# Normalising and folding the attention output of batches two and three on GpSimd instead of VectorE

## What is computed

```
attention, 4 batches, 8 heads, 576 tokens, 64 wide:
    scores = q @ k.T / 8;  kth = 32nd largest of a row
    attn = softmax(scores where scores >= kth, else -1e9)
    out = attn @ v                       # becomes x, (4, 576, 512)
first block:
    u = x + real(fft over tokens, then over width, of x)
    x = u + relu(norm(u) @ w1) @ w2      # 512 -> 2048 -> 512
second block:
    out = x + relu(norm(x) * g @ w1') @ w2'
```

## Time and profile before

| | us |
|---|---|
| median of 3 runs | 1482.75 (1481.47 to 1484.03) |
| profiled execution | 1480.5, span 1478.7 |
| PE busy | 1323.3 (89%) |
| DVE busy | 1173.6 (79%) |
| ACT busy | 670.9 (45%) |
| POOL busy | 320.0 (22%) |

### The profile page before, as it was taken

How to read it: one execution, slowest core, us unless ns; L and a number is a source line. 1 busy time by engine, 2 the same in 40 slices (tenths; PEclk the granted TensorE clock), 3 DMA queues, 4 the chain that set the end, 5 groups by cost and what they waited for, 6 DMA issues and landing times. The chain is left out here.

```text
span 1478.7 us, 22291 instructions
## 1 busy us (share of the span) xinstructions
PE 1323.3 (89%) x7944; PEld 1054.5 (71%) x7944; DVE 1173.6 (79%) x2345; ACT 670.9 (45%) x1293; POOL 320.0 (22%) x283
## 2 busy tenths in 40 slices
PE   4666768899998799899999899999998999999998
PEld 2434444677676577678877677877887989888887
DVE  7999998799999979999997999854675454555543
ACT  3555543355454335454453464433354434343432
POOL 2443420122131112131220131220123020121210
PEclk9665659999999899899999999999999999999999
DMA  6688770565565426556543454542354343333342
GB/s 209 258 301 312 282 278 9 199 209 201 197 221 185 153 91 212 181 173 195 180 158 120 167 190 150 173 144 70 116 171 140 117 147 117 127 115 123 120 139 76
DMA packets 83295, 248.61 MB, mean 168 GB/s; under 512 B 26417, under 2 KB 26418, under 8 KB 79090
## 3 DMA queue, kind: packets, MB, share of 16 engines
q1 hardware_dynamic: 81554, 241.67, 48.3%
q0 software_dynamic: 1632, 5.51, 1.1%
HBM read 208.34 MB, written 38.27 MB: 167 GB/s over the span
## 5 line engine op out<-in xcount | busy, mean ns | idle before, releaser
L580 PE MATMUL Ac<-wr,hh 128*128 128x512 f32 x1152 | 361.6, 395 | 0.0
L563 PE MATMUL Hp<-uh,wr 128*128 128x256 f32 (+1 forms) x1336 | 305.6, 319 | 7.4 <-ACT hh L763 5.0
L857 DVE MAX8 top<-wk 128x8 f32<-128x576 f32 x432 | 304.5, 746 | 0.0
L563 PEld LDWEIGHTS Hp<-uh,wr 128*128 128x128 f32 x1336 | 225.7, 193 | 55.2 <-issue 47.3
L580 PE MATMUL Ac<-wr,hl 128*128 128x512 f32 x576 | 237.9, 413 | 14.7 <-DVE wr L992 7.5
L580 PEld LDWEIGHTS Ac<-wr,hh 128*128 128x128 f32 x1152 | 218.5, 190 | 40.3
L405 POOL TENSOR_TENSOR hl<-hf,hh 128x256 fp32r<-128x256 f32 (+1 forms) x111 | 96.0, 865 | 537.4 <-ACT hh L763 537.3
L869 DVE MATCH_REPLACE8 wk<-top,wk 128x576 f32<-128x576 f32 x288 | 211.5, 741 | 0.0
L511 PE MATMUL Tp<-ident,ex 128*128 128x128 f32 x720 | 132.2, 317 | 85.4 <-DVE ex L876 81.7
L563 PE MATMUL Hp<-ul,wr 128*128 128x256 f32 (+1 forms) x668 | 206.9, 310 | 0.0
L511 PEld LDWEIGHTS Tp<-ident,ex 128*128 128x128 f32 x720 | 97.7, 162 | 127.5 <-issue 86.9
(11 more groups left out here) (118 smaller groups left out, 1724.5 us busy)
## 6 DMA issues: line engine op xcount, KB each, us to landing
wr<-w_split SPq DMA_DIRECT2D x222, 512.0 KB, 4.8
wf<-in_weights SPq DMA_DIRECT2D x89, 512.0 KB, 3.3
w_split<-wr SPq DMA_DIRECT2D x32, 1024.0 KB, 7.0
sc<-in_weights SPq DMA_DIRECT2D x56, 512.0 KB, 3.2
qT<-in_q SPq DMA_DIRECT2D x16, 288.0 KB, 4.7
kT<-in_k SPq DMA_DIRECT2D x16, 288.0 KB, 5.3
vn<-in_v SPq DMA_DIRECT2D x32, 128.0 KB, 4.9
out<-U POOLq DMA_DIRECT2D x3, 768.0 KB, 6.2
```

Source lines behind the costliest of these rows:

```text
L563: last = nc.tensor.matmul(hidden(n), a[:, kd * P:(kd + 1) * P], x[:, kd, 0:P * SIZE[p]], start=(kd == 0 and j == 0), stop=(kd == KD - 1 an ...
L580: last = nc.tensor.matmul(Ac[:, j, :], a[:, n % 2, j * P:(j + 1) * P], w, start=(f == 0 and m == 0), stop=(f == KF - 1 and m == 2))
L857: nc.vector.max(top[:, s % RING, r, :], src).then_inc(s_top, 1)
```

## The change

For batches 1 and 2 the three stages `normal_x`, `pair_x`, `fold_x` are split. DVE keeps the sums and all work on the 64-row chunk (`sums`, `fold_rest`), now after pair `18(b+1)`, one pair earlier than before. GpSimd gets the norm of the four full chunks in two halves, the two pair sums and the two folds, one of these steps in each of the slots 74 to 79 and 110 to 115, behind its own work on the unit and the turned rows and before residual adds and gains. The pieces of the transform stand two slots later (80 to 84, 116 to 120), and `combined` one pair later. PE's first piece waits for one semaphore more, `s_rem`. `late_exps` lists slots 86, 88, 90 and 122, 124, 126 instead of 74, 76, 84, 86, 88 and 110, 112, 120, 122, 124.

```diff
 def late_exps(s):
-    return s // 2 in (NT + 1, NT + 2, NT + 6, NT + 7, NT + 8, 3 * NT // 2 + 1, 3 * NT // 2 + 2, 3 * NT // 2 + 6,
-                      3 * NT // 2 + 7, 3 * NT // 2 + 8)
+    return s // 2 in (NT + 7, NT + 8, NT + 9, 3 * NT // 2 + 7, 3 * NT // 2 + 8, 3 * NT // 2 + 9)
...
-    return {1: 78, 2: 114, 3: 148}[b] + i // 2
+    return {1: 80, 2: 116, 3: 148}[b] + i // 2
...
+            def pool_normal(b, half):
+                pool.wait_ge(s_den, 4 * b + 4)
+                part = U[:, chunk(b, 2 * half):chunk(b, 2 * half) + 2, :].rearrange("p c (h d) -> p (c h) d", d=D)
+                scale = den[:, 2 * half:2 * half + 2, :].rearrange("p c h -> p (c h)").unsqueeze(2)
+                pool.tensor_tensor(part, part, scale.to_broadcast([P, 2 * H, D]), ALU.mult).then_inc(s_xn, 1)
+
+            def pool_pairs(b, side):
+                full = U[:, chunk(b, 0):chunk(b, 0) + CF, :]
+                pool.wait_ge(s_xn, 2 * b)
+                pool.wait_ge(s_comb, J * b)
+                pool.tensor_tensor(xs[:, side, :, :], full[:, 0:CF:2, :], full[:, 1:CF:2, :],
+                                   ALU.subtract if side else ALU.add).then_inc(s_pairs, 1)
+
+            def pool_fold(b, side):
+                op = ALU.subtract if side else ALU.add
+                if side:
+                    pool.memset(xf[:, :, 1, 0:1], 0.0)
+                else:
+                    pool.wait_ge(s_pairs, 2 * b + 2)
+                    pool.tensor_copy(xf[:, 0:HP, 0, 0:1], xs[:, 0, :, 0:1])
+                fold = pool.tensor_tensor(xf[:, 0:HP, side, 1:FOLD], xs[:, side, :, 1:FOLD], xs[:, side, :, DM - 1:FOLD:-1], op)
+                if side:
+                    fold.then_inc(s_fold, 1)
...
                     for t in turns_at(s):
                         un_low(t)
+                for b in (1, 2):
+                    if 0 <= s - NT * (b + 1) - 2 < 6:
+                        pool_step(b, s - NT * (b + 1) - 2)
                 for n in closing_at(s):
...
                 if i == 0:
                     pe.wait_ge(s_fold, b + 1)
+                    if b in (1, 2):
+                        pe.wait_ge(s_rem, b)
...
                 for b in (1, 2):
-                    if n == NT // 2 * (b + 1) + 1:
-                        normal_x(b)
-                    if n == NT // 2 * (b + 1) + 2:
-                        pair_x(b)
-                        fold_x(b)
+                    if n == NT // 2 * (b + 1):
+                        sums(b)
+                        fold_rest(b)
                     for j in range(J):
-                        if n == NT // 2 * (b + 1) + 6 + j:
+                        if n == NT // 2 * (b + 1) + 7 + j:
                             combined(b, j)
```

More of the change, by code:

```diff
@@ L252, in build @@
         s_pc_ps, s_pc_sb = sem("s_pc_ps"), sem("s_pc_sb")
-        s_eo, s_comb = sem("s_eo"), sem("s_comb")
+        s_eo, s_comb, s_xn, s_rem = sem("s_eo"), sem("s_comb"), sem("s_xn"), sem("s_rem")
         s_stat = [sem("s_stat0"), sem("s_stat1")]
@@ L440, in gain, with pool_step @@
                 pool.tensor_tensor(un[:, j, :], un[:, j, :], gb[:, :], ALU.mult).then_inc(s_ung, 1)
+            def pool_normal(b, half):
[19 more added lines that the diff above has]
+                    fold.then_inc(s_fold, 1)
+            def pool_step(b, i):
+                if i < 2:
+                    pool_normal(b, i)
+                if i in (2, 3):
+                    pool_pairs(b, i - 2)
+                if i >= 4:
+                    pool_fold(b, i - 4)
             def tail_rows(b):
@@ L878, in pair, with sums @@
                                                    op0=ALU.is_ge, op1=ALU.mult, accum_out=total).then_inc(s_masked, 1)
-            def normal_x(b):
-                full, rem = U[:, chunk(b, 0):chunk(b, 0) + CF, :], rest(b)
+            def sums(b):
+                rem = rest(b)
                 dve.wait_ge(s_x_sb, NT * (b + 1))
@@ L889, in normal_x, with fold_rest @@
                 nc.vector.reciprocal(den[rem, CF, :], den[rem, CF, :]).then_inc(s_den, 1)
+            def fold_rest(b):
+                rem, last = rest(b), U[rest(b), chunk(b, CF), :]
+                dve.wait_ge(s_den, 4 * b + 4)
+                nc.vector.tensor_tensor(last.rearrange("p (h d) -> p h d", d=D), xt[rem, :, 0:D],
+                                        den[rem, CF, :].unsqueeze(2).to_broadcast([TAIL, H, D]), ALU.mult).then_inc(s_norm, 1)
+                dve.wait_ge(s_norm, b + 1)
+                nc.vector.tensor_copy(xf[rem, HP, 0, 0:1], last[:, 0:1])
+                nc.vector.tensor_tensor(xf[rem, HP, 1, 1:FOLD], last[:, 1:FOLD], last[:, DM - 1:FOLD:-1], ALU.subtract)
+                nc.vector.tensor_tensor(xf[rem, HP, 0, 1:FOLD], last[:, 1:FOLD], last[:, DM - 1:FOLD:-1], ALU.add).then_inc(s_rem, 1)
+            def normal_x(b):
+                full, rem = U[:, chunk(b, 0):chunk(b, 0) + CF, :], rest(b)
+                sums(b)
                 dve.wait_ge(s_den, 4 * b + 4)
```

## The result

The changed kernel took 1472.95 us (median of four runs, 1472.01 to 1474.17) beside 1482.84 for the kernel before (four runs): ratio 0.9932, 95% interval [0.9904, 0.996]. The direction held; the gain was 9.9 us where 3.8 were forecast.

The account below looks back on a forecast made before the run. VectorE was taken to set the pace up to slot 78 and TensorE from slot 98 to 123. Second batch 2.2 plus third batch 1.6 made 3.8 us off the median 1482.75, so 1478.9; range 1474 to 1484.

Parts of the forecast that it names:

- the length of slots 76 and 77: Second batch before the pieces: 14.0 us from the old trace, plus 1.0, so slot 78 starts at 514.4 instead of 515.6.
- the late gain: Slots 76 and 77: GpSimd's pair sum delays its gain for group 3, which TensorE must turn; 1.0 us charged at slot 77.
- The charge for blocking: Slot 75: GpSimd's step runs 2.4 us across pair 38's first mask on VectorE; half charged, 1.2 us.
- the rival built on the rule: Slots 75, 77, 79: VectorE's masks or maxima wait out whole GpSimd steps, 2.4 + 2.4 + 1.3 us; about 1483; chance 0.20.
- The hidden wait: Third batch after pair 54: VectorE waits about 6 us for ScalarE's last copy of x; 1.2 us charged.
- The third batch's order: Slots 114 to 118: fewer piece slots before slot 119, the following combination counted; 2.8 us gained, before the wait's charge.
- Slot 85 came 58.5 us after slot 78: Second batch: this old distance, carried over unchanged, puts slot 85 at 572.9.
- Second batch 2.2 forecast: Pair 44 7.5 us earlier, 6.3 after late exponentials; a 4.1 us combination now behind it leaves 2.2 us gained.
- third 1.6 forecast: Third batch: 2.8 us gained from the order, less 1.2 us for VectorE's wait for the copy of x; net 1.6 us.
- GpSimd costs double: Slots 75 to 78 and third batch: GpSimd steps of 4.7 us, 5.8 us slower than before, 1488.5; chance 0.11.
- blocking eats it: Slots 75, 77, 79: masks or maxima wait out whole GpSimd steps; batches at -0.7 and 0.4 us, about 1483; chance 0.20.
- Less in the way than I charge: No mask hit, gain in time, stalled pair 55 just covered; 7.2 us off, 1475.5, or 1474.5 with TensorE's clock; chance 0.17.

Follow-up runs that it names:

- third_only: The change in the third batch alone, the second batch as in the kernel before; 1481.44 us beside 1481.09 for the kernel before, ratio 0.9994.
- pieces_only: Kernel before with only the transform pieces and combinations later and exponentials retimed, VectorE keeping its work; 1476.88 us beside 1481.09 for the kernel before.
- change_again: The change unaltered, measured in more executions; 1474.77 us beside 1481.05 for the kernel before, ratio 0.9975.
- third_pieces: The change, but in the third batch VectorE keeps norm, sums and folds and only pieces and combinations stand later; 1475.26 us beside 1481.05 for the kernel before.
- third_at_118: The change with the third batch's sums behind pair 55, pieces at slots 118 to 122, combinations one pair later; 1475.33 us beside 1481.05 for the kernel before.
- second_at_82: The change with the second batch's pieces at slots 82 to 86 and its combinations one more pair later; 1474.78 us beside 1481.05 for the kernel before.
- steps_tiny: The change with GpSimd's steps cut to a few columns, most of that work left out; 1473.68 us beside 1481.09 for the kernel before.
- sums_later: The change with the third batch's sums and 64-row fold behind pair 55 instead of 54; 1474.21 us beside 1482.3 for the kernel before.
- steps_twice: The change with each of GpSimd's steps done twice, same result; 1484.5 us beside 1482.3 for the kernel before, ratio 1.0023.
- second_only: The change in the second batch alone, the third batch as in the kernel before; 1476.54 us beside 1481.09 for the kernel before, ratio 0.998.

## Why the prediction was wrong

**The step that failed: the length of slots 76 and 77.** The prediction wrote "Slots 76 and 77 take 515.59 - 1.96 - 499.66 = 14.0 us" and carried that over. With 1.0 for the late gain it made 15.0. In the change the same two slots take 12.3 us (495.42 to 507.71), with 0.71 of waiting in them, so 11.6 of TensorE's own. The 14.0 held a low clock. Slot 74's start in the kernel before and its two stretches from there on:

```profile
482.94 0.74 PE L511 MATMUL Tp<-ident,ex 128*128 128x128 f32 x5 [2.43 <-DVE ex L876]
...
484.00:500.00 16.00, 11.00 (x72) 8.83 (x69) 15.85 (x30) 5.50 (x12) 1.64 (x2) 0.84 0.46 159
500.00:516.00 16.00, 14.04 (x91) 10.35 (x90) 15.93 (x35) 6.67 (x14) 5.22 (x5) 0.84 0.28 86
```

and of the change, from slots 74 and 76 on:

```profile
484.00:496.00 12.00, 9.94 (x75) 7.75 (x75) 11.97 (x28) 5.80 (x12) 5.18 (x4) 1.00 0.61 193
496.00:508.00 12.00, 11.29 (x87) 8.58 (x86) 11.97 (x25) 6.63 (x14) 6.89 (x6) 1.00 0.41 144
```

The granted clock is 0.84 before, part of the time at the lower level of 1.2 GHz after TensorE's waits of 2.43 and 5.00 us, and 1.00 in the change, where the waits are 0.91 and 2.06. The same eight 64-row score matmuls of slot 76 took 2.18 us before and 1.19 now:

```profile
500.89 2.18 PE L490 MATMUL Sp<-kT,qT 64*64 64x288 f32 x8
```

```profile
496.08 1.19 PE L524 MATMUL Sp<-kT,qT 64*64 64x288 f32 x8
```

With the clock up, TensorE keeps up with VectorE. Slots 72 to 77 in the kernel before and in the change, and VectorE's first mask for slot 78 in the change:

```profile
471.00:516.37 45.37, 35.89 (x239) 27.47 (x240) 45.05 (x97) 18.14 (x39) 9.25 (x11) 0.89 0.50 163
...
468.63:508.67 40.04, 33.74 (x239) 25.94 (x240) 39.77 (x89) 18.40 (x39) 15.11 (x14) 0.96 0.54 174
...
505.79 0.80 DVE L912 SCALAR_TENSOR_TENSOR ex<-sc,top,ex 128x576 f32<-128x576 f32 x1
```

VectorE is idle for only 0.3 us in both, busy 45.05 us before and 39.77 in the change, so the six slots are shorter by just what its work is shorter: 5.3 us, of the 6.0 that left it. Slot 78 itself starts by TensorE's own length: its mask was ready at 506.59, and TensorE came at 507.71. The prediction too had TensorE as the bound there, but at 15.0 us instead of 12.3, and so found 1.2 us where 4.7 to 5.4 were gained. The clock stood in the prediction, but only as a point for a rival and not in the sum.

All the profiles agree with this. In the three where VectorE keeps this work (before, third_only, pieces_only) slot 76 takes 6.2 to 6.6 us between ScalarE's copies, in the eleven others 4.6 to 4.9. In pieces_only TensorE waited 3.07 us at slot 76 instead of 5.00, and slots 76 and 77 were 0.9 us shorter in its own work; it only waited longer for the mask of slot 78 (2.78 us instead of 1.96). No run held the relief and lowered the clock of slot 76 alone, so what the clock by itself is worth there, 2.4 us, is read from the rows.

**The charge for blocking was wrong in size and place.** "The step would run some 2.4 us across pair 38's first mask; I charge half, 1.2 us." GpSimd and VectorE at that moment in the change:

```profile
491.87 1.90 POOL L445 TENSOR_TENSOR U<-U,den 128x1024 f32<-128x1024 f32 x1
```

```profile
494.46 0.80 DVE L912 SCALAR_TENSOR_TENSOR ex<-sc,top,ex 128x576 f32<-128x576 f32 x1
```

The step ends at 493.77, 0.7 us before the mask. The reason is that slot 74 too was shorter at the higher clock, so GpSimd got there sooner. That the norm took 1.90 us and not the row's 2.36 was not needed for it: with 2.36 it would have ended at 494.23, still before the mask. The clock of slot 74 is chance, and change_again, the same kernel, shows the other case. There TensorE waited 2.43 us at slot 74 instead of 0.91, the granted clock of slots 74 and 75 was 0.87, and slot 74 took 5.8 us instead of 4.2:

```profile
494.95 1.90 POOL L445 TENSOR_TENSOR U<-U,den 128x1024 f32<-128x1024 f32 x1
...
495.99 1.48 DVE L912 SCALAR_TENSOR_TENSOR ex<-sc,top,ex 128x576 f32<-128x576 f32 x1
```

The mask takes 1.48 us instead of 0.80, and slot 76 starts 0.7 us later (28.25 us after slot 72 instead of 27.56). third_pieces, third_at_118 and second_at_82 show the same. steps_tiny has the low clock in slot 74 too, but no step there, and starts slot 76 at 27.56. So blocking costs 0 or 0.7 us at this place, not 1.2. TensorE starts slot 76 1.9 us earlier in the change and 1.2 in change_again, counted from slot 72, where 0.3 were forecast. One slot later another operation of GpSimd, the low part of the turned rows, holds up the second mask of pair 39, and behind it a step holds up the small scaling:

```profile
506.13 1.61 POOL L411 TENSOR_TENSOR ul<-uf,uh 128x512 fp32r<-128x512 f32 x1 [1.07 <-ACT uf L789]
507.70 2.89 POOL L451 TENSOR_TENSOR xs<-U 128x1024 f32<-128x1024 f32 x1
```

```profile
506.51 1.84 DVE L912 SCALAR_TENSOR_TENSOR ex<-sc,top,ex 128x576 f32<-128x576 f32 x1
509.73 0.89 DVE L900 TENSOR_SCALAR nmx<-top 128x2 f32<-128x2 f32 x1
```

The small scaling ends at 510.62, with GpSimd's sum at 510.59. With the rule of the Trainium skill (SBUF — State Buffer, Who interferes with whom), that the later one waits until the earlier has finished, the trace agrees. GpSimd's sum in turn waited for the mask, and took 2.89 us instead of 2.38. The mask and the scaling cost VectorE 1.0 and 0.7 us, which the prediction did not have; with them the rival built on the rule was right about the mechanism and wrong about how often and where.

**Right, with sizes.** The late gain: charged 1.0 us, 0.71 at slot 77 and another 1.00 at slot 78; steps_tiny shows that all of GpSimd's steps together cost the second batch some 2 us. Pair 44 starts 2.2 us after slot 85, where 2.1 were forecast. The hidden wait: forecast a wait of about 6 us and a cost of 1.2; measured 6.41 us idle and 0.9, taken back by sums_later. The third batch's order: forecast 2.8, measured 2.6 to 2.7 in pieces_only and third_pieces, where VectorE keeps its work.

**Wrong, and smaller.** "Slot 85 came 58.5 us after slot 78", carried over, is 60.1 in the change: the 1.00 us for the gain at slot 78 and 0.60 for the mask at slot 80 stand in it. Pair 44 starts 9.9 us earlier than before, counted from slot 72, where 7.5 were forecast, since slot 78 is earlier. From slot 78 to 98 nothing changes in the sum (140.5 us in both), where the prediction's working gave 1.0. The third batch came out at 2.5 us where 1.6 were forecast: 0.3 is the cheaper hidden wait, and the change gives 0.6 to 0.8 more behind slot 110 than the order alone, which is no more than the scatter of that column.

**The sum.** Second batch 2.2 forecast, 4.8 to 5.4 measured; third 1.6 forecast, 2.5 measured; 3.8 against about 7. The mechanisms were in the main the right ones, and the term for slots 72 to 78 was mis-sized. The rival "GpSimd costs double" forecast 5.8 us slower than before; steps_twice, with steps of twice the length, is 2.2 slower by the medians, with an interval that covers both 5.8 and nothing, and about 5 by the stages of its one profiled execution. The stages split this 2 and 3, where the rival had 5.0 and 0.8. The rival "blocking eats it" did not come about. "Less in the way than I charge" has the number: 1475.5, or 1474.5 with TensorE's clock, beside the later median of 1474.77. The clock that it named came; its conditions did not: in the change one mask is held up (1.84 us), the gain is late by 0.71 and 1.00, and the stalled pair 55 costs 0.9. With those the number fits by luck.

## What to carry to other kernels

A duration read behind a wait of TensorE may hold the lower clock; before carrying it into a changed schedule, look at the same instructions in another slot at full clock (here 1.19 against 2.18 us) and make the sum with both. Moving a pause behind independent work can gain time without any engine being relieved, here 2.6 us where TensorE was the bound before it and little where VectorE was: try the order alone before moving work. And work given to a slower engine pays only as long as it fits the room in its queue: here at 2 us a step it did, at 4 the whole gain was gone.

## What the runs showed that I had not expected

Slot 37, the transform of the first batch, changes its length from execution to execution, in code that no kernel here changes: 24.1 us in most profiles, 25.9, 27.4, and 38.1 once. Busy time by stretch of that slot in the change, in second_only and in steps_twice:

```profile
229.00:253.00 24.00, 22.11 (x92) 11.39 (x94) 21.12 (x47) 7.16 (x17) 1.06 (x2) 0.95 0.00 1
```

```profile
229.00:257.00 28.00, 24.84 (x95) 11.98 (x94) 21.89 (x48) 7.74 (x17) 1.05 (x2) 0.88 0.00 1
```

```profile
229.00:267.00 38.00, 35.43 (x92) 16.14 (x92) 22.44 (x49) 7.33 (x16) 0.92 (x2) 0.58 0.00 1
```

The granted clock is 0.95, 0.88 and 0.58, the work the same. Before this slot TensorE has been waiting for VectorE in every pair, 4.08 us at slot 36 in the change. What decides when the clock rises there was not tried; it was worth 14 us of this kernel in one execution, more than the change, and that execution of steps_twice was 14.3 us over its median.

And on GpSimd the product with a repeated operand, 128x1024, took 1.90 to 1.91 us undisturbed, where a sum of two full operands of that size took 2.38 to 2.39. That this is the repeated operand and not the product is likely but was not tried: at 128x512 the gain's product of two full operands and the difference for the turned rows both take 1.29 us in the median.
